# Attention with two MLP layers: the softmax scaling moves from GpSimd to ScalarE and VectorE, and the first two chunks' steps and units are placed anew

## The reference, cut to what matters

```python
B, H, S, D = 4, 8, 576, 64
scores = q @ k.T / 8                          # per batch and head, 576 x 576
kth = 32nd largest of each row
scores = where(scores >= kth, scores, -1e9)
attn = exp(scores - max(scores));  attn = attn / (sum(attn) + 1e-9)
x = (attn @ v)                                # heads side by side: 2304 tokens x 512
h = x @ w_in (512 x 2048);  g = max(0.01 h, h);  x = g @ w_out (2048 x 512)
h = x @ w_in2;  g = where(h >= 1, h, where(h <= -1, 0, (h + 1)**2 / 4));  out = g @ w_out2
```

## Time and profile before

| what | us |
|---|---|
| runs | 1191.25, 1191.4, 1193.39 (median 1191.4) |
| profiled execution | 1196.05 |
| its span | 1194.0 |
| mean granted clock | 0.973 |

### The profile page before, as it was taken

One profiled execution on the slowest core, in us unless ns is written; L12 is line 12 of the kernel. 1 busy time (PEld: TensorE's weight loads), 2 busy tenths in 40 slices (PEclk: granted clock), 3 DMA queues, 4 the chain that ended last, 5 costly groups with the idle time before them and its releaser, 6 DMA issues.

```text
span 1194.0 us, 20896 instructions
## 1 busy us (share of the span) xinstructions
PE 1112.1 (93%) x7360; PEld 1005.9 (84%) x7360; DVE 867.7 (73%) x2088; ACT 709.3 (59%) x1595; POOL 617.8 (52%) x566
## 2 busy tenths in 40 slices
PE   4457998899999999999999989999999999999998
PEld 2336887788989888889988978898889999999998
DVE  7999978878799887898978978969988006300234
ACT  6887777656577665666666756666765324312232
POOL 5435779835377554665446744545855423222222
PEclk9868998989999999999999989999999999999999
DMA  8888987775667787767666747545456577787664
GB/s 286 294 322 296 360 301 296 249 246 198 236 204 254 233 284 257 260 245 249 237 238 213 252 147 244 177 166 187 145 192 225 200 254 247 262 275 255 249 237 150
DMA packets 86790, 287.10 MB, mean 240 GB/s; under 512 B 9632, under 2 KB 13472, under 8 KB 86688
## 3 DMA queue, kind: packets, MB, share of 16 engines
q1 hardware_dynamic: 79200, 270.04, 65.2%
q10 hardware_dynamic: 7488, 15.73, 3.9%
HBM read 247.46 MB, written 38.27 MB: 239 GB/s over the span
## 4 chain that ended last, share of the span: by engine, by line
PE 79%; DVE 10%; ACT 4%; POOL 4%; issue 2%; DMA 1%; POOLq 0%; ACTq 0%; SPq 0%; DVEq 0%
PE ps_f L812 21%; PE ps_f L820 20%; PE ps_f L813 20%; PE ps_av L771 6%; DVE top L1077 5%; DVE work L1080 4%; PE ps_s L724 3%; PE ps_t L748 2%; PE ps_t L724 2%; PE ps_t L754 2%; POOL probs L628 1%; POOL w_ring L621 1%; PE ps_s L730 1%; DMA raw<-wd 1%; DVE part_r L1104 1%
## 5 line engine op out<-in xcount | busy, mean ns | idle before, releaser
L1077 DVE MAX8 top<-work 128x8 f32<-128x576 f32 x432 | 310.0, 744 | 0.1
L812 PE MATMUL ps_f<-xy,w_ring 128*128 128x384 f32 (+2 forms) x896 | 289.4, 323 | 1.5 <-ACT xy L999 1.5
L812 PE MATMUL ps_f<-gate,w_ring 128*128 128x384 f32 (+2 forms) x896 | 287.3, 321 | 1.2 <-ACT gate L992 1.2
L820 PE MATMUL ps_f<-gate,w_ring 128*128 128x384 f32 (+2 forms) x896 | 282.4, 315 | 5.4 <-POOL gate L643 5.3
L820 PE MATMUL ps_f<-xy,w_ring 128*128 128x384 f32 (+2 forms) x896 | 281.6, 314 | 1.3 <-POOL xy L653 1.2
L813 PE MATMUL ps_f<-xy,w_ring 128*128 128x384 f32 (+2 forms) x896 | 281.1, 314 | 0.0
L813 PE MATMUL ps_f<-gate,w_ring 128*128 128x384 f32 (+2 forms) x896 | 281.0, 314 | 0.0
L628 POOL TENSOR_SCALAR probs<-probs,row_inv 128x576 f32<-128x576 f32 x128 | 222.2, 1747 | 106.8 <-DVE row_inv L1098 106.8
L1080 DVE MATCH_REPLACE8 work<-top,work 128x576 f32<-128x576 f32 x288 | 213.5, 741 | 0.0
L812 PEld LDWEIGHTS ps_f<-xy,w_ring 128*128 128x128 f32 x896 | 170.5, 190 | 16.7 <-issue 8.9
L643 POOL TENSOR_TENSOR gate<-part_r,gate 128x384 fp32r<-128x384 f32 (+2 forms) x112 | 100.2, 899 | 160.2 <-ACT gate L984 159.8
(11 more groups left out here) (83 smaller groups left out, 1784.7 us busy)
## 6 DMA issues: line engine op xcount, KB each, us to landing
w_ring<-w_split SPq DMA_DIRECT2D x412, 512.0 KB, 4.2
w_split<-w_ring SPq DMA_DIRECT2D x36, 512.0 KB, 6.4
raw<-wd SPq DMA_DIRECT2D x64, 256.0 KB, 5.2
w_split<-xy SPq DMA_DIRECT2D x28, 512.0 KB, 4.4
kq<-kqd ACTq DMA_DIRECT2D x12, 576.0 KB, 5.7
v_sb<-vd ACTq DMA_DIRECT2D x12, 320.0 KB, 3.9
out_t<-y_acc ACTq DMA_DIRECT2D x12, 192.0 KB, 3.9
kq<-kqd SPq DMA_DIRECT2D x3, 576.0 KB, 6.7
```

Source lines behind the costliest of these rows:

```text
L812: pe.matmul(out, w[:, 0, m], high, start=first, stop=False)
L820: mm = pe.matmul(out, w[:, 0, m], low, start=False, stop=end)
L1077: dve.max(top[:, t % T_SLOTS, 8 * r:8 * r + 8], source(t, r)).then_inc(dve_step, 1)
```

## The change

It has five parts. (1) The first chunk's items are transposed at last + 5 instead of last + 6; `keep` and `exponential` run at t + 4 until `READY[0]`, which becomes 21; DVE closes those items' sums in the middle of iteration last + 2. (2) Scaling: ACT scales the first tile of every item, in 72 of them at the step before the transposes; the second tile is scaled by POOL for items 0 to 6 (a TENSOR_TENSOR with a broadcast operand, at the start of the step) and by DVE for every other item that has one, right after `invert_sum`. (3) The pair gp = 7, the second chunk's last (items 17 to 19), is `hurried`: closed one iteration sooner, exponentiated at t + 4, transposed at last + 6, its values and x at the end of that same step; `READY[1]` becomes 42. (4) The planner decides what leads a block's outputs only when they are due, so that the next block's or chunk's first hidden units stand between a block's last hidden unit and its outputs; `FIRST_FILL` becomes 3797 (so that 0.1.1's outputs are left over for step 42), `FILL` 4275. (5) Scores are not put at the head of a step if the step before ended with transposes.

```diff
+FIRST_EXP_LAG = 4
-FILL = 4350.0
+FILL = 4275.0
+def hurried(gp):
+    return gp == CHUNKS[1].last_gp
 def out_step(it):
-    return it.last + (6 if starts_early(it.gp) else 7)
+    return it.last + (5 if starts_early(it.gp) else 6 if hurried(it.gp) else 7)
 def values_step(gp):
-    return out_step(last) + (not starts_early(gp))
+    return out_step(last) + (not starts_early(gp) and not hurried(gp))
-FIRST_FILL = FIRST_NS / (READY[1] - READY[0])
+FIRST_FILL = (FIRST_NS - CK * BLOCK_F * PRODUCTS * (CHUNKS[0].width / 2.4 + 12)) / (READY[1] - READY[0])
...
         while True:
-            if not queue and at < len(order) and READY[order[at][0].n] <= s:
+            if not queue and outputs:
+                if credit < outputs[0].ns / 2 and s < ATTENTION_STEPS:
+                    break
+                if at < len(order):
+                    nc, nlayer, nblock = order[at]
+                    if nblock or (not nlayer and READY[nc.n] <= s):
+                        led = lead(nc)
+                        queue = segment(nc, nlayer, nblock, True, range(led))
+                queue, outputs = queue + outputs, []
+            elif not queue and at < len(order) and READY[order[at][0].n] <= s:
                 c, layer, block = order[at]
                 queue = segment(c, layer, block, True, range(led, BLOCK_F))
+                outputs = segment(c, layer, block, False, range(CK))
                 led, at = 0, at + 1
-                (the lead and the outputs were queued here)
...
 def scores_first(s):
-    return s in OUT_AT
+    return s in OUT_AT and not (s - 1 in OUT_AT and not PLAN[s - 1][2])
+def by_pool(it):
+    return starts_early(it.gp) and it.last < FIRST_END
+def by_dve(it):
+    return not it.mixed and not by_pool(it)
...
             # POOL, at the start of step s, for OUT_AT[s] if by_pool
             def normalise(it):
                 pool.wait_ge(inv_ready, it.n + 1)
-                for a in range(it.tiles):
-                    p = probs[:, it.n % P_SLOTS, a * S:(a + 1) * S]
-                    op = pool.tensor_scalar(p, p, row_inv[:, it.n % T_SLOTS, a:a + 1], None, ALU.mult)
-                op.then_inc(probs_ready_late, 1)
+                p = probs[:, it.n % P_SLOTS, S:2 * S]
+                pool.tensor_tensor(p, p, row_inv[:, it.n % T_SLOTS, 1:2].to_broadcast([P, S]),
+                                   ALU.mult).then_inc(probs_ready_pool, 1)
...
             # PE: transpose(it) waits for ACT's part, and POOL's or DVE's
+                pe.wait_ge(probs_ready, it.n + 1)
+                if by_pool(it):
+                    pe.wait_ge(probs_ready_pool, scaled(by_pool, it))
+                elif by_dve(it):
+                    pe.wait_ge(probs_ready_dve, scaled(by_dve, it))
...
             # ACT
             def normalise(it):
                 act.wait_ge(inv_ready, it.n + 1)
-                for a in range(it.tiles):
-                    p = probs[:, it.n % P_SLOTS, a * S:(a + 1) * S]
-                    op = act.activation(p, p, ACT.Copy, scale=row_inv[:, it.n % T_SLOTS, a:a + 1])
-                op.then_inc(probs_ready, 1)
+                p = probs[:, it.n % P_SLOTS, 0:S]
+                act.activation(p, p, ACT.Copy, scale=row_inv[:, it.n % T_SLOTS, 0:1]).then_inc(probs_ready, 1)
...
                 if not scores_first(s):
                     for it in SCORED_AT[s]:
                         copy_scores(it)
+                if s + 1 in OUT_AT:
+                    normalise(OUT_AT[s + 1])
+                if soon is not None:
+                    keep(soon)
                 for u in second:
                     event(u)
+                if soon is not None:
+                    exponential(soon)
...
             # DVE
+            def normalise(it):
+                dve.wait_ge(inv_ready, it.n + 1)
+                p = probs[:, it.n % P_SLOTS, S:2 * S]
+                dve.tensor_scalar(p, p, row_inv[:, it.n % T_SLOTS, 1:2], None, ALU.mult).then_inc(probs_ready_dve, 1)
...
+                if early:
+                    close_sum(shut)
                 if new:
                     dve.wait_ge(dve_step, first_drop)
                     top8(t, 1)
+                if early:
+                    dve.wait_ge(dve_step, closed)
+                    invert_sum(shut)
...
-                if shut:
+                if late:
                     dve.wait_ge(dve_step, count)
                     invert_sum(shut)
+                    if by_dve(shut):
+                        normalise(shut)
```

More of the change, by code:

```diff
@@ L389, in item_closing @@
             continue
-        if it.last + INV_LAG - starts_early(it.gp) == t:
+        if it.last + INV_LAG - (starts_early(it.gp) or hurried(it.gp)) == t:
             return it
@@ L405, with exp_tile, hurried_tile, scaled @@
 ITEMS_SCORED = [sum(score_step(o) <= out_step(it) for o in ITEMS) for it in ITEMS]
+def exp_tile(s):
+    if s == READY[0] - 1:
+        return None
+    t = s - (FIRST_EXP_LAG if s < READY[0] else EXP_LAG)
+    return t if 0 <= t < TILES and not hurried(ITEM_OF[t].gp) else None
+def hurried_tile(s):
+    t = s - EXP_LAG + 1
+    return t if s >= READY[0] and t < TILES and hurried(ITEM_OF[t].gp) else None
+def by_pool(it):
+    return starts_early(it.gp) and it.last < FIRST_END
+def by_dve(it):
+    return not it.mixed and not by_pool(it)
+def scaled(kind, it):
+    return sum(kind(o) for o in ITEMS[:it.n + 1])
 def need(eng, sem, value):
@@ L685, in _ @@
             for s, (first, second, third) in enumerate(PLAN):
+                if s in OUT_AT and by_pool(OUT_AT[s]):
+                    normalise(OUT_AT[s])
                 if s == READY[0] - 2:
@@ L699, in _ @@
                     event(u)
-                if s + 1 in OUT_AT and not starts_early(OUT_AT[s + 1].gp):
-                    normalise(OUT_AT[s + 1])
                 for u in second:
                     event(u)
-                if s in VALUES_AT and s >= READY[0]:
+                if s in VALUES_AT and s >= READY[0] and not hurried(VALUES_AT[s]):
                     low_x(VALUES_AT[s])
@@ L707, in _ @@
                     event(u)
+                if s in VALUES_AT and hurried(VALUES_AT[s]):
+                    low_x(VALUES_AT[s])
         @block.tensor
@@ L858, in _ @@
                         score(it)
-                if s in VALUES_AT:
+                if s in VALUES_AT and not hurried(VALUES_AT[s]):
                     values(VALUES_AT[s])
@@ L866, in _ @@
                     feed(u)
+                if s in VALUES_AT and hurried(VALUES_AT[s]):
+                    values(VALUES_AT[s])
         @block.scalar
@@ L1020, in _ @@
                         copy_transposed(done)
-                    elif s >= EXP_LAG:
-                        keep(s - EXP_LAG)
                     if s - 1 in OUT_AT:
                         copy_transposed(OUT_AT[s - 1])
-                    if EXP_LAG <= s < READY[0] - 1:
-                        exponential(s - EXP_LAG)
+                    if t is not None:
+                        keep(t)
                     for it in SCORED_AT[s]:
                         copy_scores(it)
+                    if t is not None:
+                        exponential(t)
                     if s - 2 in VALUES_AT:
@@ L1040, in _ @@
                     copy_values(CHUNKS[0].last_gp)
-                    keep(s - 1 - EXP_LAG)
-                elif s < TILES + EXP_LAG:
-                    keep(s - EXP_LAG)
+                if t is not None:
+                    keep(t)
                 for u in first:
                     event(u)
-                if s == READY[0]:
-                    exponential(s - 1 - EXP_LAG)
-                elif s < TILES + EXP_LAG:
-                    exponential(s - EXP_LAG)
+                if t is not None:
+                    exponential(t)
                 if not scores_first(s):
@@ L1062, in _ @@
                     event(u)
-                if s == READY[0]:
-                    exponential(s - EXP_LAG)
+                if s in VALUES_AT and hurried(VALUES_AT[s]):
+                    copy_values(VALUES_AT[s])
             while to_finish:
@@ L1140, in _ @@
                 shut = item_closing(t)
+                early = shut is not None and starts_early(shut.gp)
+                late = shut is not None and not early
                 before = count
```

31 lines of the change are left out of this document (11 added, 20 removed).

## The result

| | before | after |
|---|---|---|
| runs, median us | 1191.7 (1191.25 to 1193.39) | 1182.93 (1182.27 to 1184.15) |
| profiled execution | 1196.05 | 1182.27 |
| its span | 1194.0 | 1180.5 |
| mean granted clock | 0.973 | 0.977 |

The medians are of four runs each; 1196.05 is not among the four of before, 1182.27 is one of the four of after. The ratio is 0.9913, with a 95% interval of 0.9897 to 0.9929: 8.8 us faster. The forecast was 28.8 us and 1163, its range 1152 to 1181. The sign was right; the time lies outside the range.

A forecast was written before the change was run, and what follows sets the result against it. PE was taken as the bound, savings counting only where it stands idle or slow. Four terms, 2.0 + 2.0 + 12.8 + 12.0 = 28.8 us, came off a median of 1191.4 to give 1163, range 1152 to 1181.

The forecast's parts named there:

- 5.97 against PE's 4.275 + 2.0 = 6.28, so it is hidden: DVE's 57 added scalings, 0.6 us each, 0.3 a step: DVE's average step stays below PE's, so they cost nothing.
- DVE takes POOL's place in the chain: Rival: DVE's layer-1 iterations set the pace and early closes make it wait; gain only 14 us, 1177; chance 0.18.
- First term: First chunk, up to 105 us: earlier close of item sums and less ACT scaling save 2.0 us, bounds 0 to 3.
- the estimate of 93.45 for the close: First chunk: DVE closes the sum after tile 15's bounds at 93.45 instead of 94.80, 1.35 us sooner.
- Second term: Steps 21 to 23: shorter PE wait for ACT's score copy and less low clock save 2.0 us, bounds 0 to 3.3.
- Third term: 180 to 260 us: POOL's scaling no longer causes transpose and gate waits; saves 12.8 us, bounds 8 to 16.3.
- Fourth term: 260 to 900 us: transpose, gate and p_rem waits and a low-clock place go; saves 12.0 us, bounds 0 to 15.5.
- The median of the runs is 4.6 below the profiled execution: Conversion from profile to runs: before's median taken as 1191.4 against 1196.05 profiled, then 28.8 subtracted to give 1163.
- ACT waits for `row_inv`: Rival: ACT waits for DVE's inverse ahead of bank reads and PE's banks fill; 14 us if all paid, 1177; chance 0.10.
- DVE and POOL lock one another out: Rival: DVE scalings costing 1.16 us or more make DVE the bound from step 42; up to 1202; chance 0.07.
- `READY[1]` at 0: FILL and READY[1] only move units between steps while PE's total stays, so they were costed at 0.
- The signs set for being wrong: DVE scalings above 1.1 us, PE waits for ACT ending at row_inv or bounds, or steps 33 to 42 over 6.5 each.

The follow-up runs named there:

- best: after, with later items' second tiles on POOL, steps ended between a unit and one waiting for it, first-chunk sums closed at iteration's end: 1166.70 us, ratio 0.9785.
- old_first: after, with the first chunk's steps as before (READY[0] = 22, transposes at last + 6, sums closed at the end, ACT scaling both tiles): 1188.79 us, ratio 0.9970.
- scale_only: before, with only the later items' scaling moved from POOL to ACT (first tile) and DVE (second tile): 1187.98 us, ratio 0.9958.
- pool_second: after, with the second tile of every later whole item scaled by POOL instead of DVE: 1170.86 us, ratio 0.9810.
- before_again: the kernel before, unchanged, profiled a second time: 1195.9 us, one run; before's median on that chip 1193.23.
- no_hurry: after, with pair gp = 7 not hurried and READY[1] = 44 (FIRST_FILL 3467): 1186.62 us, ratio 0.9942.

## Why the prediction was wrong

**The failed step** is "5.97 against PE's 4.275 + 2.0 = 6.28, so it is hidden". Two averages were compared. By DVE's rows in after, iterations 46 to 141 hold 5.84 us of work in the mean, but 4.99 to 7.68 singly, and 22 of the 96 hold more than 6.28. Those with a `y_acc` hold 6.1 in the mean, those with curves alone 5.8. PE's steps are uneven too: by the plan the units of one are 2.8 to 7.0 us. What counts is where PE waits at the end of a chain through DVE, as at step 81, and there a scaling costs its whole duration. The 35 us that were called hidden cost 12 (1182.9 to 1170.9); of the 7.0 that the terms had taken off for DVE's pace and new waits, 2.7 were scaling (0.3 in each of nine steps). With the second tiles on POOL the profiled gain is 26.1 of the forecast 28.8; by the ratio, 0.9810, it is 22.6.

The rival "DVE takes POOL's place in the chain" named this mechanism and gave it 0.18. Its sum of 14 us is near the 13.5 of the spans, but by luck: its parts were 0, 1, 8 and 5, the measured ones -0.3, 2.9, 2.5 and 8.4, and its time of 1177 is 6 below the median.

**The range.** Besides, the range was narrower than its own terms. Their lower bounds are 0, 0, 8 and 0, so 8 us and not "20 at least"; their upper ones add up to 38.1, not 37. A range from these bounds would have ended at 1183.4 and held the measured 1182.93.

**First term, 2.0, measured -0.3.** The measured value has the spread of 3 us named above. The prediction named the middle-of-iteration close as a cost of "its lateness" and took none. DVE and ACT after, around item 7:

```profile
92.98 0.20 DVE L1128 TENSOR_SCALAR bounds<-top 128x1 f32<-128x1 f32 x1
...
96.95 0.17 DVE L1134 TENSOR_SCALAR row_eps<-row_sum 128x2 f32<-128x2 f32 x1 [1.45 <-ACT probs L963]
...
97.35 0.52 DVE L1144 TENSOR_SCALAR probs<-probs,row_inv 128x576 f32<-128x576 f32 x1
```
```profile
94.16 1.03 ACT L976 ACTIVATE p_t<-ps_t 128x1024 f32<-128x1024 f32 x1 [0.32 <-PE ps_av L795]
...
95.24 0.78 ACT L955 ACTIVATE probs<-scores,bounds 128x576 f32<-128x576 f32 x1
```

Tile 15's bounds are ready 2.9 us later than in the earlier trace rows. From them to the close it takes 3.8 instead of 4.5. Nor does a close at the end of the iteration bring all of the 2.0. In best the bounds are back at 90.49, but ACT's copy of item 6's transposes, now ahead of `keep(15)`, waits for PE until 93.53, and DVE waits 3.50 for the close:

```profile
96.31 0.17 DVE L1138 TENSOR_SCALAR row_eps<-row_sum 128x2 f32<-128x2 f32 x1 [3.50 <-ACT probs L967]
```

The step missed here is that a copy moved ahead of `keep` brings along its wait for the transposes; the estimate of 93.45 for the close had only its duration.

**Second term, 2.0, measured 2.9**: right in kind, and within its bounds. From 105 to 120 PE's idle time went from 2.0 to 0.65 and the clock from 0.89 to 1.00. About half of it needs no change of the first chunk: in old_first the same stretch is 1.5 shorter than before.

**Third term, 12.8, measured 2.5.** POOL's part was right for the transposes: the wait of 4.9 is 1.7. It was wrong for the gates, as scale_only shows. But PE met new waits, 0.97 and 1.00 at 171 and 173, 2.28 for `p_rem` at 210.6, 0.96 at 217.3, each with low clock around it (0.97 and 0.98 in the two stretches). The prediction had put 3.5 to DVE here; with DVE relieved the term is 8.2, so DVE took 5.7 and waits that are no matter of DVE's scaling the other 4.6 (in pool_second PE still waits 1.67 at 195 and 1.76 at 207). Ahead of the wait at 210.6 in after, ACT has no gap from 205.3 on, and a scaling of 0.78 is part of that work. ACT went from 51.3 to 63.0 us of the 80 there, so its share of the scaling, costed at nothing as well, may have its part in these waits; no run took it away.

**Fourth term, 12.0, measured 8.4**, and 15.8 with DVE relieved: without the load the forecast for this part would have been too low. Of the waits the turns of layers are the main kind; keeping them apart brought 4.7 us by the medians.

**From the profile to the median.** "The median of the runs is 4.6 below the profiled execution" was carried over to the changed kernel as a constant. It holds for before (again in before_again, by 3 to 5) and not for after, where the profiled execution is 0.7 below the median. This alone is 4.7 us of the 20 by which the forecast missed, and a second step that failed. Why before's profiled executions are longer was not tried.

**The other rivals.** "ACT waits for `row_inv`" fell: 13 waits, 10.3 us from 120 to 930, forecast below 15, and none of PE's longer waits ends there. "DVE and POOL lock one another out" is a real mechanism here at a small price (below): the mean scaling is 0.617, far from the 1.16 at which it would decide. `READY[1]` at 0 was probably too low: in no_hurry the pair's two steps, with the credit that goes with them, are worth 2.4 to 3.7, near the limit of what the runs tell.

**The signs that were named.** Of what the profile after would show, POOL's busy time (408) and DVE's (899) came near 410 and 905. Three signs of a lesser gain were there. PE is idle 14.6 us from 180 to 900 instead of below 8, the mean clock is 0.977 and not above 0.98, and item 7's transposes begin at 98.18 (before 96.70, forecast 94.7). The signs set for being wrong didn't appear: the mean scaling on DVE is 0.617 and not above 1.1, no long wait of PE ends at `row_inv` or `bounds`, and DVE's iterations for steps 33 to 42 take 6.27 each, below 6.5. They looked for a lasting pace, and the loss came at single places.

## What to carry to other kernels

Work moved off a stalling engine isn't hidden on the next one because its average per step fits under TensorE's. Look at the steps in which that engine feeds a result that TensorE needs (here `y_acc` to `xy`), and count the whole duration there. Here the engine that had slack only on average was the worst receiver, and one that is slower per instruction was the better one: 65 us on POOL cost less than 35 us on DVE. Add up the bounds of the terms before the range is written down. And compare a profiled execution with a profiled one: its distance to the median was 4.7 us for one kernel here and below 1 for the other.

## What the runs showed of the hardware

**A broadcast operand is the faster scaling on POOL.** TENSOR_SCALAR of 128x576 took 1747 ns in before; TENSOR_TENSOR with the row's factor broadcast took 1148 ns in after and, in pool_second:

```profile
L665 POOL TENSOR_TENSOR probs<-probs,row_inv 128x576 f32<-128x576 f32 x63 | 72.9, 1157 | 122.6 <-DVE row_inv L1141 122.6
```

**DVE's scaling waits out POOL's TENSOR_TENSOR.** Of the 57 in after, 39 ran with POOL idle and took 0.52 us each. Fourteen began while a POOL TENSOR_TENSOR ran (one of them 0.01 ahead of it), took 0.63 to 1.24, and every one ended 0.31 or 0.32 us behind the end of that instruction, as at 279.55 below (DVE ends at 280.76, POOL's at 280.44). Of the other four, which began just ahead of POOL's, the one with a lead of 0.03 us took 1.07 and three with 0.09 to 0.23 took 0.52. The case at 279.55:

```profile
279.55 1.21 DVE L1144 TENSOR_SCALAR probs<-probs,row_inv 128x576 f32<-128x576 f32 x1
```
```profile
279.56 0.88 POOL L680 TENSOR_TENSOR gate<-part_r,gate 128x320 fp32r<-128x320 f32 x1 [1.85 <-ACT gate L1024]
```

The small close does the same (54.16 above), and in before the L1093 at 76.22 ends at 77.27, two of POOL's from 74.75 for 2.50 at 77.25. Single MAX8 and MATCH_REPLACE8 stay at 0.73 to 0.76 throughout this trace. In all this cost DVE 5.6 us (35.2 less 57 x 0.52). The Trainium skill (SBUF — State Buffer, "SBUF: two separate sides") has such a lock for the port pair that both engines share, on VectorE's side for operations in a two-port mode or with two inputs in SBUF. The trace agrees for these instructions. For the undisturbed 0.52 the Trainium skill (VectorE: DVE Perf Modes, "Mode 2×_2P — use both read ports for one tensor") led to an estimate of 0.4: the measurement is 0.12 above it.
